# Attention inside a three-layer kernel: the inverse's Z tiles in two sets with a first product of half the width, scaled keys in halves, new orders of the steps, and eleven more products of a cleared tile

## The reference

```python
k_n = k / (np.linalg.norm(k, axis=-1, keepdims=True) + 1e-06)
state = np.zeros((B, H, D, D), dtype=np.float32)
for t in range(S):
    kt, vt, bt = (k_n[:, :, t], v[:, :, t], beta[:, :, t, None])
    y[:, :, t] = np.einsum('bhd,bhde->bhe', q[:, :, t], state)
    v_old = np.einsum('bhde,bhd->bhe', state, kt)
    state = state + bt[:, :, :, None] * np.einsum('bhd,bhe->bhde', kt, vt - v_old)
```

## Time and profile before

| | us |
|---|---|
| median of 3 runs | 2361.82 (2361.77 to 2361.85) |
| the profiled execution's own time | 2361.32 |
| its span, first to last instruction | 2359.5 |
| mean granted TensorE clock | 0.998 |

### The profile page before, as it was taken

One profiled execution on the slowest core, in us unless ns is written; L12 is line 12 of the kernel. 1 busy time (PEld: TensorE's weight loads), 2 busy tenths in 40 slices (PEclk: granted clock), 3 DMA queues, 4 the chain that ended last, 5 costly groups with the idle time before them and its releaser, 6 DMA issues.

```text
span 2359.5 us, 38749 instructions
## 1 busy us (share of the span) xinstructions
PE 2341.0 (99%) x15924; PEld 1960.6 (83%) x15924; DVE 1281.0 (54%) x2496; ACT 838.2 (36%) x1865; POOL 385.9 (16%) x318
## 2 busy tenths in 40 slices
PE   8999999999999999999999999999999999999999
PEld 7899988888888788888888888888888888888887
DVE  7888888877777463334343343433433434334344
ACT  6888887666666311111111111111111111111111
POOL 6777762000000000000000000000000000000000
PEclk9999999999999999999999999999999999999999
DMA  3222222100000101101011010110101101011013
GB/s 95 52 58 61 50 48 56 41 0 0 0 0 28 35 1 56 41 14 45 10 54 41 14 48 7 54 41 14 50 5 54 41 14 50 9 50 43 16 35 68
DMA packets 101298, 82.29 MB, mean 35 GB/s; under 512 B 75136, under 2 KB 82048, under 8 KB 99200
## 3 DMA queue, kind: packets, MB, share of 16 engines
q1 hardware_dynamic: 100992, 79.79, 11.5%
q10 hardware_dynamic: 144, 0.20, 0.0%
HBM read 74.95 MB, written 8.16 MB: 35 GB/s over the span
## 4 chain that ended last, share of the span: by engine, by line
PE 93%; DVE 5%; issue 1%; ACT 0%; DMA 0%; POOL 0%; SPq 0%; DVEq 0%; ACTq 0%
PE ex_h L160 46%; PE ex_y L160 45%; PE ex_logits L160 2%; DVE at_X L569 1%; DVE at_gram L512 1%; DVE de_w_lo L908 1%; DVE de_en L923 1%; DVE de_hg L936 1%; PE ex_y L629 0%; DVE de_g_lo L916 0%; DVE at_gram L514 0%; DVE de_en L921 0%; DMA at_k_in<-k 0%; DVE at_Z L572 0%; DVE at_gram L559 0%
## 5 line engine op out<-in xcount | busy, mean ns | idle before, releaser
L1372 DVE SCALAR_TENSOR_TENSOR ex_r_lo<-ex_h,ex_r_hi 128x512 fp32r<-128x512 f32 x384 | 264.3, 688 | 928.5 <-ACT ex_r_hi L1249 928.1
L1249 ACT ACTIVATE ex_r_hi<-ex_h 128x512 fp32r<-128x512 f32 x384 | 229.8, 599 | 1283.8 <-PE ex_h L160 1283.8
L160 PE MATMUL ex_h<-x_hi,ex_w_lo 128*128 128x512 f32 x1152 | 448.7, 389 | 0.0
L160 PE MATMUL ex_h<-x_hi,ex_w_hi 128*128 128x512 f32 x1152 | 448.7, 389 | 0.0
L160 PE MATMUL ex_h<-x_lo,ex_w_hi 128*128 128x512 f32 x1152 | 448.5, 389 | 0.0
L160 PE MATMUL ex_y<-ex_r_lo,ex_w_hi 128*128 128x512 f32 x1152 | 448.2, 389 | 0.0
L160 PE MATMUL ex_y<-ex_r_hi,ex_w_lo 128*128 128x512 f32 x1152 | 448.2, 389 | 0.0
L160 PE MATMUL ex_y<-ex_r_hi,ex_w_hi 128*128 128x512 f32 x1152 | 448.1, 389 | 0.0
L1199 POOL TENSOR_TENSOR ex_w_lo<-ex_stage,ex_w_hi 128x512 fp32r<-128x512 f32 x90 | 115.7, 1287 | 1674.6 <-ACT ex_w_hi L1231 1636.5
L160 PEld LDWEIGHTS ex_h<-x_hi,ex_w_hi 128*128 128x128 f32 x1152 | 216.3, 188 | 45.1 <-issue 0.2
L160 PEld LDWEIGHTS ex_h<-x_hi,ex_w_lo 128*128 128x128 f32 x1152 | 216.3, 188 | 44.9
(11 more groups left out here) (188 smaller groups left out, 3209.5 us busy)
## 6 DMA issues: line engine op xcount, KB each, us to landing
ex_stage<-w_exp SPq DMA_DIRECT2D x15, 1536.0 KB, 6.4
ex_pb<-p_rows SPq DMA_DIRECT2D x90, 256.0 KB, 3.3
at_qT<-q_t SPq DMA_DIRECT2D x12, 512.0 KB, 3.6
at_k_in<-k SPq DMA_DIRECT2D x12, 384.0 KB, 3.2
out<-ex_stage SPq DMA_DIRECT2D x60, 64.0 KB, 1.9
de_stage<-w_rows SPq DMA_DIRECT2D x8, 384.0 KB, 3.2
de_stage<-w_out SPq DMA_DIRECT2D x8, 384.0 KB, 3.2
at_v_in<-v SPq DMA_DIRECT2D x12, 192.0 KB, 3.7
```

The costliest lines, as they stand in the source:

```text
L160: return nc.tensor.matmul(out, lhsT, rhs, start=start, stop=stop)
L1249: nc.scalar.activation(r[0][:, j, :], h_bank[j][:], ACT.Relu).then_inc(hi_ready, 1)
L1372: nc.vector.scalar_tensor_tensor(out=r[1][:, j, :], in0=h_bank[j][:], scalar=0.0, in1=r[0][:, j, :].bitcast(F32), op0=ALU.max, op1=ALU.sub ...
```

## The change

**Z in two sets.** The tiles `Z2` go; `Z` becomes `Z[w][g]`, one set for even and one for odd waves. `ZZ` writes its masked tile straight into `Z[w][g]`, and `Z0` updates only the changed half in place, as the later `Z` steps do: four products of 64 columns in place of 128, and a copy of 256 columns in place of 512. `ZZ` no longer waits for the previous wave's `Z0`; on POOL it waits for the `corr` of two waves earlier.

**Scaled keys in halves.** `knh.0` and `knh.1` replace `kn` in every wave, both on POOL (the first wave's `knh.0` stays on DVE). Each has a semaphore of its own, so `F1.0` waits for eight heads only. The halves wait for two `B4` steps each.

**The added 1e-6** moves from DVE's `inv` to ACT's `sqrt`, as a second small instruction. In wave 0 the squares are split 6 heads on POOL to 10 on DVE instead of 8 to 8.

**A cleared tile's products.** The 12 at the start become 10, and eleven `warm` steps of one such product each are put between the first steps of wave 0 (into the bank of group 3).

**All orders are written anew.** Groups 0 and 1 now lead, and 2 and 3 follow.

```diff
-WARM_UP = 12
+WARM_UP = 10
...
-    Z2 = tiles("Z2_", range(91, 95), [P, 4, P], F16)
-    Z = tiles("Z", range(121, 125), [P, 4, P], F16)
+    Z = [tiles("Z0_", range(91, 95), [P, 4, P], F16), tiles("Z1_", range(121, 125), [P, 4, P], F16)]
...
+    SPLIT = [slice(10, UH), slice(0, 10)]
...
-        return tile[:, j, :] if step == ("Z", 0) else pair_half(step[1], step[0] == "Z", tile)[:, j]
+        return pair_half(step[1], step[0] == "Z", tile)[:, j]
...
             if kind == "knh":
                 pool.wait_ge(rnorm, n + 1)
+                if n >= W:
+                    for x in (2 * g, 2 * g + 1):
+                        filled(pool, "B4", x, n - W)
                 nc.gpsimd.tensor_tensor(kn[w][:, HALF[g], 0:D], k_in[w][:, HALF[g]], by_norm(n)[:, HALF[g]],
-                                        ALU.mult).then_inc(scaled, 1)
+                                        ALU.mult).then_inc(scaled[g], 1)
...
             if kind == "ZZ":
                 pool.wait_ge(NT_ready[g], n + 1)
-                if n > 0:
-                    pool.wait_ge(M_filled[g], m_count(n - 1, ("Z", 0)))
-                nc.gpsimd.tensor_tensor(Z2[g][:], NT[w][g][:], four(z2mask), ALU.mult).then_inc(Z2_ready[g], 1)
+                if n >= W:
+                    pool.wait_ge(M_drained[g], m_count(n - W, "corr"))
+                nc.gpsimd.tensor_tensor(Z[w][g][:], NT[w][g][:], four(z2mask), ALU.mult).then_inc(Z2_ready[g], 1)
...
                 nc.scalar.activation(norm[w][:, 1, :], norm[w][:, 0, :], ACT.Sqrt).then_inc(rooted, 1)
+                act.wait_ge(rooted, n + 1)
+                nc.scalar.activation(norm[w][:, 2, :], norm[w][:, 1, :], ACT.Copy, bias=1e-6).then_inc(biased, 1)
...
-                pe.wait_ge(scaled, 2 * (n + 1))
+                pe.wait_ge(scaled[g], n + 1)
...
+            elif kind == "warm":
+                mm(nc, M_bank[G - 1][:, 0:2 * P], zeros[:, 0:P], zeros)
...
 ATTENTION_ROUND = {
...
     "POOL": (
-        "ZZ.3@-2 RT.1@-2 RT.0@-2 kn@-1 RT.3@-2 RT.2@-2 NT.2@-1 NT.1@-1 ZZ.1@-1 NT.0@-1 sq@+1 ZZ.0@-1 ZZ.2@-1 "
-        "NT.3@-1 "),
+        "RT.1@-2 ZZ.2@-2 NT.3@-2 ZZ.3@-2 sq RT.0@-2 RT.2@-2 knh.0@-1 RT.3@-2 knh.1@-1 NT.0@-1 ZZ.0@-1 NT.1@-1 "
+        "ZZ.1@-1 NT.2@-1 "),
```

More of the change, by code:

```diff
@@ L227, in attention_programs @@
     loaded_q = [s.sem(f"loaded_q{w}") for w in range(W)]
-    squared, summed, rooted, biased, rnorm, scaled = s.sems("squared summed rooted biased rnorm scaled")
+    squared, summed, rooted, biased, rnorm = s.sems("squared summed rooted biased rnorm")
+    scaled = [s.sem(f"scaled{u}") for u in range(2)]
     rest_ready, hn_ready = s.sems("rest_ready hn_ready")
@@ L327, in merged @@
     def merged(step, bank):
-        if step == ("Z", 0):
-            return bank4(bank)
         return bank[:, 0:4 * (P // 2)].rearrange("p (f b c) -> p f b c", f=4, c=MERGES[step[1]])
@@ L376, in sp_program @@
             if kind == "loadk" and n >= W:
-                sp.wait_ge(scaled, 2 * (n - W + 1))
+                for u in range(2):
+                    sp.wait_ge(scaled[u], n - W + 1)
                 load_k(sp, n)
@@ L394, in pool_program @@
                 pool.wait_ge(loaded_k[w], 16 * (c + 1))
[L395 to L396 removed]
+                nc.gpsimd.tensor_tensor(square[:, SPLIT[g]], k_in[w][:, SPLIT[g]], k_in[w][:, SPLIT[g]], ALU.mult).then_inc(squared, 1)
+            if kind == "knh":
                 pool.wait_ge(rnorm, n + 1)
                 if n >= W:
[L399 removed]
+                    for x in (2 * g, 2 * g + 1):
                         filled(pool, "B4", x, n - W)
[L401 to L403 removed]
                 nc.gpsimd.tensor_tensor(kn[w][:, HALF[g], 0:D], k_in[w][:, HALF[g]], by_norm(n)[:, HALF[g]],
[L405 removed]
+                                        ALU.mult).then_inc(scaled[g], 1)
             if kind == "NT":
@@ L465, in step @@
                 else:
-                    to = (T if at[0] == "T" else Z)[g]
+                    to = T[g] if at[0] == "T" else Z[w][g]
                     nc.scalar.copy(changed(at, to), merged(at, M_bank[g])).then_inc(M_drained[g], 1)
@@ L522, in step @@
                 dve.wait_ge(NT_ready[g], n + 1)
[L523 to L525 removed]
+                nc.vector.tensor_tensor(Z[w][g][:], NT[w][g][:], four(z2mask), ALU.mult).then_inc(Z2_ready[g], 1)
             elif kind == "R":
@@ L571, in step @@
                 else:
-                    nc.vector.tensor_copy(changed(at, (T if at[0] == "T" else Z)[g]),
+                    nc.vector.tensor_copy(changed(at, T[g] if at[0] == "T" else Z[w][g]),
                                           merged(at, M_bank[g])).then_inc(M_drained[g], 1)
@@ L601, in merge @@
                 pe.wait_ge(RT_ready[g], n + 1)
-            z = Z2[g] if at in ("T2", ("T", 0), ("Z", 0)) else Z[g]
+            z = Z[w][g]
             for j in range(4):
@@ L733, in attention_programs @@
     first_h = [O_bank[o_bank(f"h{f}", 0, NW - 1)] for f in range(BEGUN)]
-    return Attention(sp_program, pool_program, act_program, dve_program, pe_program, kn_read, (scaled, 2 * NW),
+    return Attention(sp_program, pool_program, act_program, dve_program, pe_program, kn_read, [(scaled[u], NW) for u in range(2)],
                      [(O_drained[o_bank("Q", u, NW - 1)], o_count("Q", u, NW - 1)) for u in range(2)], first_h, hn_ready,
@@ L893, in fill @@
             if kind == "split":
-                act.wait_ge(*attention.k_read)
+                for read in attention.k_read:
+                    act.wait_ge(*read)
                 split(f)
```

24 lines of the change are left out of this document (5 added, 19 removed), and 159 rows, old and new, of tables (ATTENTION_HEAD, ATTENTION_LAST, ATTENTION_ROUND).

## The result

The changed kernel takes 2348.43 us (median of 4 runs, 2347.76 to 2348.82) against 2361.8 us before: ratio 0.9944, 95% interval 0.9929 to 0.9958, so 13.4 us less where 14.4 were forecast. The profiled execution took 2348.05 us.

What follows compares the result with a forecast made beforehand. PE's issue was taken to bound 27.3 of 30.5 us a steady wave, DVE 3.2. Gains of 9.4 (ten waves) + 3 (start) + 2 (end) = 14.4 us gave 2347.4 us; own range 2339 to 2356, eight in ten 2336 to 2358.

Steps and rivals of the forecast that it cites:

- the sum for a steady wave: Steady attention waves: 0.42 + 0.82 - 0.30 = 0.94 us less each, 9.4 us over ten of the twelve waves.
- The start: Wave 0: earlier `F1.0` and first `eX`, about 2 us, plus 1 us from the clock; 3 us, bounds 0 and 6.
- the end: End of attention: earlier `h1` removes two PE waits, 1.9 us, and fills waiting time; 2 us taken, bounds 0 and 4.
- PE's 0.42: `Z0` at half width: PE saves 0.10 us for each of four groups, about 0.42 us a wave, on the chain.
- I count that as nothing: `Z0`'s shorter copy on ACT saves 0.85 us a wave, counted as zero because ACT has idle time.
- I take all of it off that stall: Moving the 1e-6 off DVE takes 0.82 us a wave off DVE's second stall of 1.66 us; bounds 0 and 0.82.
- The stall at `F1.1`: PE waits for POOL's second half of the scaled keys: 0.3 us a wave lost, bounds 0 and 0.6.
- No gain and no loss: The new orders by themselves change nothing; 1.5 us a wave kept for the range either way.
- The first: Rival: the orders also dissolve one of two DVE stalls, 1.5 us a wave more, time 2332; chance 0.14.
- The second: Rival: steady waves gain nothing, only start and end remain, about 2358 us; chance 0.10.
- POOL is not the bound: Answers a rival: POOL becomes the bound, deciding from 7.3 us a wave of waits for `gram`; 2369 us, chance 0.07.
- The clock term: Wave 0: cleared products fill PE's idle time and keep the clock from halving, worth 1 us.

Runs made afterwards that it cites:

- e2: Changed kernel with the 1e-6 back on DVE and `Z0` at full width; new orders, cleared products and halves stay: 2354.30 us, ratio 0.9969.
- e6: Changed kernel with the products of `Z0` at 128 columns again, its copy still half: 2351.36 us, ratio 0.9957.
- e4: Changed kernel with `Z0` at full width again, both products and copy: 2354.14 us, ratio 0.9968.
- e3: Changed kernel with the addition of 1e-6 back on DVE, nothing else undone: 2349.04 us, ratio 0.9946.
- e5: Kernel before the change with one edit, the addition of 1e-6 moved from DVE to ACT: 2362.57 us, ratio 1.0005.
- e12: Changed kernel with each half of the scaled keys on POOL in three instructions from wave 2 on: 2349.22 us, ratio 0.9946.
- e9: Changed kernel with the scaled keys whole, one POOL instruction from wave 3 on where the first half stood: 2359.38 us, ratio 0.9991.
- e1: Changed kernel's new parts under the order tables of the kernel before, with twelve first products: 2359.76 us, ratio 0.9992.
- e10: Changed kernel with the four `gram` steps in the middle of DVE's round placed one behind the other: 2371.10 us, ratio 1.0039.
- e11: Changed kernel with twelve first products of the cleared tile instead of ten: 2349.13 us, ratio 0.9946.
- e7: Changed kernel without the eleven cleared products among wave 0's steps; ten first products stay: 2348.75 us, ratio 0.9946.
- e8: Changed kernel with `h1` moved behind the last wave's `W.1` and `g.1` behind the last `xhi` and `xlo`: 2351.08 us, ratio 0.9957.

## Why the prediction was right, and where its steps were not

The time was right to 1 us, and that was in good part luck: the sum for a steady wave, 0.42 + 0.82 - 0.30 = 0.94 us, came out by errors that cancel, and so did the sum of the stretches. The start brought 1.9 us where 3 were forecast, waves 2 to 11 brought 7.3 where 9.4 were (8.7 less the 1.4 by which wave 11 grew), and the end 4.2 where 2 were. Measured for a steady wave are 0.92 us, on one path of undoing the parts: 0.39 from the new orders with the halves (e2), 0.30 from PE's narrower `Z0` (e6), 0.22 from its shorter copy (e4 less e6), 0.01 from the addition (e2 less e4; e3 and e5 show none).

*`Z0`.* The mechanism was right; PE's 0.42 (by its own rows 4 x 0.10 = 0.40) measures 0.30. "I count that as nothing" of ACT's copy failed: 0.22 us a wave. ACT's idle time did not cover a copy for which the group's next step on PE waits.

*The 1e-6.* "I take all of it off that stall" is the step that failed, worth 0.82 us in the forecast and nothing in the steady waves of two runs. The bound named there, 0, was the truth. A gap-free stretch of DVE ahead of a stall did not mean that it would move up as a whole; behind the addition stood a `gram` that could not start before PE's `F2`. Nor were the 0.82 us work of the addition: most of it was a wait for POOL (last section).

*The stall at `F1.1`.* It never came. Its price was wrong (1.20 us from wave 0, where DVE was in the way as the last section shows, and 0.829 in steady waves), and so was its count: at 1.12 us there is still none (e12). The Trainium skill (GPSIMD Engine Reference, 3.1 Elementwise) gave some 0.83 us for a half, which the trace bears out at this length. It doesn't bear out the whole: at the same rate 768 elements would take 1.66 us, and 1.475 are measured.

*The new orders.* "No gain and no loss" failed, by 0.39 us a wave. The count of close pairs of merge steps, 11 of 84 in either order, told nothing about it. In the new order without the halves the wave would be longer than before even with the narrow `Z0` (e9, 30.83 against 30.47), so order and halves have to be taken as one edit (with Z in two sets, which no run undoes); under the old orders the parts together bring 0.29 (e1), of which the addition is nothing (e5). What in the orders brings the 0.39 stays open. In the waits of PE 0.26 of it shows (7.4 less 5.1 us, by nine), which is hardly more than that view's own unevenness, and e10 met a bank instead.

*The rivals.* The first, 1.5 us a wave more from a stall that dissolves, had half its mechanism right: PE's waits for `eX` and `eZ` are gone. Its price could not be, since by the view of waits PE had stood still for only 0.8 to 1.0 us a wave because of DVE. For the other 2.2 to 2.4 us of DVE on the chain that view shows no wait of PE. The second, that the steady waves gain nothing, is out by 8.7 us. POOL is not the bound: its waits for `gram` are 3.86 and 1.31 us a wave, 5.2 and not the 7.3 from which it would decide.

*The start.* 1.9 of 3 us. 1.2 of it lie before `F1.0`: 0.8 from two first products fewer (e11 beside e10) and the rest from the chance moment at which these products turn cheaper. The forecast took their mean of 0.66 us for each of the two; the last ones cost 0.43. Behind `F1.0` are the other 0.65 (71.06 less 70.41 us). The cleared products give 0.8 there (e7), so the rest of the new head order brings nothing there or loses 0.2, if the two add. The forecast's 2 us for an earlier `F1.0` and a better order measure 1.0: the first `eX` did come 3.2 us earlier, and most of that was lost again by wave 1's end. The clock term, 1 us, was of the right size.

*The end.* 4.2 less the 1.4 us by which the last wave grew is 2.8, where 2 were forecast; the place of `h1` alone is worth 2.65 (e8). Of that 1.7 is the two waits (1.11 + 0.8 less the 0.2 left); the rest would be the part of `h1` that now fills holes. Of the 1.4 us `h1` is 0.5 (e8). The other 0.8 came with the new order of the last wave, which the forecast had counted among its ten gaining ones; no run looked into it.

No run here beats the changed kernel; e7 lies 0.3 us above it, inside what can be told apart.

## What to carry to other kernels

Before a stall on another engine is priced from the chain of waits, look up in the waits of the bounding engine how long it really stood still: that, here 0.8 to 1.0 and not 3.2 us a wave, is about what relief can bring. Before an instruction is counted as gained on an engine, ask what the next one behind it waits for; a transfer of 0.82 us between engines bought nothing because the next input was 0.6 us away. An instruction that takes its input in one piece waits for the last part of it: cutting POOL's into halves, which cost it 12% more time in sum, was worth 1.3 us a wave in this order, mostly by what each half no longer waits for. And a difference of under 1 us at the start of a trace can be chance; count from an event behind it that all traces share.
